# Linear attention and two gated layers on one core: idle-time products in the first batch, a second numerator buffer, split denominators, and output tiles shared between two engines

## The chip, the cores and the metric

The kernel runs on one core of a Trainium2 chip. The metric is the device time of one execution in microseconds (us), so smaller is better. Engines are named as in the profile: PE is TensorE (PEld its weight loads), DVE VectorE, ACT ScalarE, POOL GpSimd, SP SyncE, which here only issues DMAs. Each runs its own list of instructions in order and waits on semaphores for the others.

## What is computed

Inputs are 8 batches of 8 heads with 576 tokens and 64 dimensions. Attention is linear, with a feature map made of two exponentials; two token-wise layers follow.

```python
def phi(x):
    proj = np.einsum('bhsd,df->bhsf', x, w_phi)                 # 64 -> 128
    proj = proj - np.max(np.abs(proj), axis=-1, keepdims=True)
    return np.concatenate([np.exp(proj), np.exp(-proj)], axis=-1)
q_p, k_p = (phi(q), phi(k))
kv = np.einsum('bhsf,bhsd->bhfd', k_p, v)
z = np.sum(k_p, axis=2)
x = np.einsum('bhsf,bhfd->bhsd', q_p, kv) / (np.einsum('bhsf,bhf->bhs', q_p, z)[..., None] + 1e-06)
...
k = np.maximum(xk @ w_k, 0.0)          # xk, xr: x mixed with the token before, 512 -> 1024
y = 1.0 / (1.0 + np.exp(-(xr @ w_r))) * (k * k @ w_v)
...
h = np.maximum(y @ w_in, 0.0)          # 512 -> 1024, then a 3-tap convolution over tokens
out = (h * (1.0 / (1.0 + np.exp(-conv_out))) @ w_out)
```

## The kernel before

**Phase 1** does the attention and the first layer. Heads go in four pairs per batch, numbered p = 0 to 3. The first batch has nothing to run beside it: its order is written out in `first_attention_steps()`. From then on `iteration(batch)` weaves the attention of the next batch into the first layer's products of this one (tiles K, R, V in `psm`, three products for one at full precision, from a high and a low part of both operands). The steps of a pair, which every engine walks through in the same order and takes its own share of, are:

- `G` and `F`: PE projects keys into `ps1` and queries into `ps0` or `psm` (p even or odd); DVE then takes the key maxima and subtracts them (lines 948 to 961).
- `QT`: DVE transposes the projected queries and reduces them to partial maxima `q_part` (lines 966 to 973). `M`: PE turns them (line 640), DVE spreads them to `max_blocks` (977 to 985). `PICK`: PE subtracts them, ACT takes the four exponentials `q_exp` (line 837).
- `EK`, `EL`: ACT takes the exponentials of the keys (826, 830). `KV0`, `KV1`: PE sums keys by values, 9 float32 products each with 65 or 130 columns; ACT copies them to `kvz` (856).
- `DEN`, `NUM`: PE forms denominators and numerators. For pairs 0 and 1 ACT copies the denominators to `den_rows` (861) and the numerators to `num` (871). The denominators go through DMAs: out to `den_parts`, inverted by DVE on 9 columns (991, 994), stored to `den_scr`, read back to `den` by all partitions. `DV`: DVE multiplies `num` by `den` into `x` (1000). For pairs 2 and 3 (`WIDE` = 2) PE writes the denominator on all rows, ACT copies both to `num_first` and `den_first` (865, 866), and DVE inverts and multiplies half the tokens at a time (`D0`, `D1`, lines 1006 and 1009).
- `SH`, `SL`: one of ten weight pieces is rounded by ACT (line 820), and POOL takes what is left of it (line 554), a DMA having loaded it into `diff`, `mix` or `gate`. `XK`, `HK`, `LK`: DVE mixes tokens and splits the result for the first K tiles (1026 to 1053).

There is one `num` buffer, so `copy_num` of pair 1 waits until DVE has used that of pair 0 (`await_x`), and PE's projection of queries for pair 3, which goes over the same bank in PSUM, waits for `copy_num` of pair 1 (`await_q_psum`).

At the start, before data is there, PE runs `keep_warm(WARM_FIRST)`: 7 products of the identity with itself, written to an unused part of `ps1`. The step `WARM`, which does the same with `WARM` products, exists but no list contains it.

**Phase 2** does the second layer, batch by batch, two batches making a round c with half 0 and 1. PE makes 8 hidden tiles in `psh` (24 products each, 288 columns a product), then output tiles of 128 tokens by 512 columns: tiles 0 to 3 in `pso` (96 products for a batch), and after half 1 a tile 4 with the last 64 tokens of both batches, in the bank `psh[:, 1, 1]` (24 products). ACT scales each by 0.5 into `rows` (line 1254), and SP stores them (1172 to 1176). The semaphore `rows_ready` counts ACT's copies; PE and SP wait on it. At the end SP waits for all stores.

## Time and profile before

| | us |
|---|---|
| median of 3 timed runs | 1289.95 (1288.88 to 1289.97) |
| profiled execution | 1286.36 |
| its span in the profile | 1284.6 |
| PE busy | 1265.4 (99% of the span) |
| DVE, ACT, POOL busy | 816.4, 563.1, 142.8 |

Times in the rows count from the start of the span. A matmul in float32 shows as two records. A number in brackets is the idle time of that engine before the row, with what ended it. The granted TensorE clock stands as a share of full speed: 1.00 is 2.4 GHz, 0.50 is 1.2 GHz.

### The profile page before, as it was taken

Reading aid. Unit: us, or ns where it says so; the run is one execution under the profiler, and the core shown is the slowest. Engines: PE = TensorE matmul, PEld = TensorE weight load, DVE = VectorE, ACT = ScalarE, POOL = GpSimd, SP = SyncE. Lnnn points to the kernel's source line nnn. Section 1 sums busy time; section 2 is a strip of 40 time slices with the busy share of each in tenths; the row PEclk is TensorE's granted clock in tenths of the full one; section 3 lists DMA queues with packets and bytes.
Section 4 is the critical chain, followed back from the end, with each engine's and each line's share of the span. In section 5 each row is a group of like instructions: output and inputs, shape, how many; then the busy total and the mean of one; then the engine's idle time right before and its main releaser. Section 6 shows DMA issues by size and latency. Waiting matters only on the chain.

```text
span 1284.6 us, 23638 instructions
## 1 busy us (share of the span) xinstructions
PE 1265.4 (99%) x9506; PEld 1081.3 (84%) x9506; DVE 816.4 (64%) x1334; ACT 563.1 (44%) x1072; POOL 142.8 (11%) x137
## 2 busy tenths in 40 slices
PE   8889999999999999999999999999999999999998
PEld 6668887888788879788878878999899898898996
DVE  6788576576566766667657666546484583672852
ACT  4653634525434354353443544454344353352441
POOL 2512111102111211121111211000000000000000
PEclk8999999999999999999999999999999999999999
DMA  5512211221222222222131220422102102012001
GB/s 163 163 40 74 65 49 47 83 68 31 79 59 60 61 57 59 69 59 59 41 88 39 60 78 12 134 70 68 70 1 79 48 23 78 1 70 79 1 34 41
DMA packets 91540, 79.03 MB, mean 62 GB/s; under 512 B 61864, under 2 KB 70184, under 8 KB 90408
## 3 DMA queue, kind: packets, MB, share of 16 engines
q1 hardware_dynamic: 91272, 77.46, 19.9%
q8 instruction: 76, 1.25, 0.4%
q14 instruction: 32, 0.26, 0.1%
q10 hardware_dynamic: 160, 0.07, 0.0%
HBM read 58.21 MB, written 19.01 MB: 60 GB/s over the span
## 4 chain that ended last, share of the span: by engine, by line
PE 90%; DVE 3%; issue 3%; DMA 2%; ACT 1%; SPq 0%; ACTq 0%; DVEq 0%
PE psm L574 36%; PE ps L574 22%; PE psh L1197 6%; PE psh L1198 6%; PE psh L1196 6%; PE pso L1198 5%; PE pso L1196 5%; PE pso L1197 5%; PE ps L686 1%; DMA den<-den_scr 1%; ACT k_signs L826 1%; DMA den_scr<-den_cols 1%; DVE q_part L969 0%; DMA phi<-in_w_phi 0%; DVE mix L1034 0%
## 5 line engine op out<-in xcount | busy, mean ns | idle before, releaser
L574 PE MATMUL psm<-xy_hi,wk_hi 128*128 128x288 f32 x512 | 156.4, 306 | 6.6 <-DVE xy_lo L1053 3.9
L574 PE MATMUL psm<-k_hi,wv_hi 128*128 128x288 f32 x512 | 153.8, 300 | 0.0
L1198 PE MATMUL psh<-xy_hi,win_lo 128*128 128x288 f32 x512 | 151.3, 296 | 0.0
L1196 PE MATMUL psh<-xy_hi,win_hi 128*128 128x288 f32 x512 | 151.3, 296 | 0.0
L1197 PE MATMUL psh<-xy_lo,win_hi 128*128 128x288 f32 x512 | 151.3, 296 | 0.0
L574 PE MATMUL psm<-xy_lo,wk_hi 128*128 128x288 f32 x512 | 151.1, 295 | 0.0
L574 PE MATMUL psm<-k_lo,wv_hi 128*128 128x288 f32 x512 | 150.9, 295 | 0.0
L574 PE MATMUL psm<-k_hi,wv_lo 128*128 128x288 f32 x512 | 150.8, 295 | 0.0
L574 PE MATMUL psm<-xy_hi,wk_lo 128*128 128x288 f32 x512 | 150.7, 294 | 0.0
L1320 DVE SCALAR_TENSOR_TENSOR conv<-h,taps,conv 128x576 f32<-128x576 f32 x64 | 52.1, 814 | 138.8 <-ACT conv L1275 138.8
L562 POOL TENSOR_TENSOR z_pairs<-k_signs 128x512 f32<-128x512 f32 x56 | 73.2, 1307 | 601.7 <-ACT k_signs L826 597.7
L1058 DVE TENSOR_TENSOR k_lo<-square,k_hi 128x288 fp32r<-128x288 f32 x128 | 76.1, 617 | 62.4 <-ACT square L881 61.7
L826 ACT ACTIVATE k_signs<-k_signs 128x1152 f32<-128x1152 f32 x32 | 37.2, 1164 | 156.3 <-issue 138.8
L574 PEld LDWEIGHTS psm<-xy_hi,wk_hi 128*128 128x128 f32 x512 | 96.1, 188 | 10.9 <-ACT relu L876 4.0
L1198 PE MATMUL pso<-wk_hi,g_lo 128*128 128x512 f32 x256 | 101.3, 396 | 0.0
L1196 PE MATMUL pso<-wk_hi,g_hi 128*128 128x512 f32 x256 | 101.3, 396 | 0.0
L1197 PE MATMUL pso<-wk_lo,g_hi 128*128 128x512 f32 x256 | 101.2, 395 | 0.0
L574 PE MATMUL ps<-q_exp,kvz 128*64 128x512 f32 (+2 forms) x960 | 100.1, 415 | 0.0
L574 PEld LDWEIGHTS psm<-k_hi,wv_hi 128*128 128x128 f32 x512 | 96.2, 188 | 1.8
L1197 PEld LDWEIGHTS psh<-xy_lo,win_hi 128*128 128x128 f32 x512 | 96.3, 188 | 0.3
L1196 PEld LDWEIGHTS psh<-xy_hi,win_hi 128*128 128x128 f32 x512 | 96.1, 188 | 0.3
L574 PEld LDWEIGHTS psm<-xy_lo,wk_hi 128*128 128x128 f32 x512 | 96.3, 188 | 0.0
(147 smaller groups left out, 2830.2 us busy)
## 6 DMA issues: line engine op xcount, KB each, us to landing
k_in<-in_k SPq DMA_DIRECT2D x32, 320.0 KB, 3.3
v_nat<-in_v SPq DMA_DIRECT2D x32, 320.0 KB, 3.6
q_in<-in_q SPq DMA_DIRECT2D x32, 288.0 KB, 3.1
y_scr<-y SPq DMA_DIRECT2D x64, 144.0 KB, 2.5
y<-y_scr SPq DMA_DIRECT2D x8, 1152.0 KB, 5.8
den<-den_scr SPq DMA_DIRECT2D x60, 144.0 KB, 3.0
out<-rows SPq DMA_DIRECT2D x32, 256.0 KB, 2.0
stage<-in_moe_w_in SPq DMA_DIRECT2D x4, 512.0 KB, 4.0
```

The lines of the kernel that those rows point to most:

```text
L562: nc.gpsimd.tensor_tensor(z_pairs[:], tiles[:, 0], tiles[:, 1], ALU.add).then_inc(z_paired, 1)
L574: return nc.tensor.matmul(o, lhsT, rhs, start=first, stop=last, skip_group_check=True)
L686: last = nc.tensor.matmul(sums_back()[:, i, :], kvt[:, i, :], ident[:], start=True, stop=True, is_transpose=True, skip_group_check=True)
L826: nc.scalar.activation(k_exp, k_shift, ACT.Exp).then_inc(k_exp_ready, 1)
L1058: nc.vector.tensor_tensor(k2_lo[:, i, :], square[:, i % 2, :], k2_hi[:, i, :].bitcast(F32), ALU.subtract).then_inc(k2_lo_ready, 1)
L1196: nc.tensor.matmul(o, wh, xh, start=first, stop=False, skip_group_check=True)
L1197: nc.tensor.matmul(o, wh, xl, start=False, stop=False, skip_group_check=True)
L1198: return nc.tensor.matmul(o, wl, xh, start=False, stop=last, skip_group_check=True)
L1320: nc.vector.scalar_tensor_tensor(out=conv[:, j % 2, :], in0=h[:, hidden(c, half, j) % 3, 0:S], scalar=taps[:, 0, j:j + 1], in1=conv[:, j % ...
```

## The change

In the first batch, `WARM_FIRST` goes from 7 to 8, and a step `WARM` with 4 products is put ahead of `KV0` of pair 0. The numerators of pair 1 of the first batch go to `square`, a buffer of the first layer, so that their copy doesn't wait for `x`. `copy_wide` copies the first half of the denominators, then the numerators, then the second half. In phase 2, DVE takes the output tiles 1 and 3 (a new `copy_rows`), ACT keeps 0, 2 and 4, and `rows_ready` becomes `even_rows` and `odd_rows`. In the last round only, tile 4 is computed, copied and stored as two halves of 256 columns, each in a bank of its own.

```diff
-WARM_FIRST, WARM = 7, 6
+WARM_FIRST, WARM = 8, 4
...
-    steps = [("G", 0), ("F", 0), ("EK", 0), ("F", 1), ("QT", 0), ("KV0", 0), ("M", 0)] + hi()
+    steps = [("G", 0), ("F", 0), ("EK", 0), ("F", 1), ("QT", 0), ("WARM", 0), ("KV0", 0), ("M", 0)] + hi()
...
+    def numerator(p, a):
+
+        return square[:].rearrange("p i s -> p (i s)") if (p, a) == (1, 0) else num[:]
...
+            nc.scalar.activation(den_first[:, p - WIDE, 0:HALF], q_cols(1, p, a)[:, 0:HALF], ACT.Copy, bias=1e-6).then_inc(first_den, 1)
             nc.scalar.activation(num_first[:, p - WIDE, :], q_cols(0, p, a), ACT.Copy).then_inc(num_copied, 1)
-            nc.scalar.activation(den_first[:, p - WIDE, :], q_cols(1, p, a), ACT.Copy, bias=1e-6).then_inc(first_den, 1)
+            nc.scalar.activation(den_first[:, p - WIDE, HALF:S], q_cols(1, p, a)[:, HALF:S], ACT.Copy, bias=1e-6).then_inc(first_den, 1)
...
-            await_x(act, p, a)
-            nc.scalar.activation(num[:], q_cols(0, p, a), ACT.Copy).then_inc(num_copied, 1)
+            if (p, a) != (1, 0):
+                await_x(act, p, a)
+            nc.scalar.activation(numerator(p, a), q_cols(0, p, a), ACT.Copy).then_inc(num_copied, 1)
...
-            dve.wait_ge(first_den, own + 1)
+            dve.wait_ge(first_den, 2 * own + n + 1)
...
+    def await_all_rows(eng, c, half):
+
+        eng.wait_ge(even_rows, 5 * c + 2 * half)
+        eng.wait_ge(odd_rows, 4 * c + 2 * half)
+
+    def last_columns(c):
+
+        halves = slice(0, DM // 2), slice(DM // 2, DM)
+        return halves if c == TWOS - 1 else (slice(0, DM),)
...
-                for j in range(FT):
-                    last = out_part(0, 4, j)
-                last.then_inc(out_done, 1)
+                for n, cols in enumerate(last_columns(c)):
+                    for j in range(FT):
+                        last = out_part(0, 4, j, cols, n)
+                    last.then_inc(out_done, 1)
...
-            for t in range(4 + half):
+            for t in range(0, 4 + half, 2):
                 copy_rows(c, half, t)
...
+            for t in (1, 3):
+                copy_rows(c, half, t)
```

PE in the first batch, pair 0, before: query projections of pair 1 (`psm`), then `KV0`, then `M`.

```order
L574 MATMUL psm<-q_in,phi 128x64 [waits shared_bank] x2
L574 MATMUL ps<-v_nat,k_signs 128x65 [waits k_exp_ready,v_loaded]
L574 MATMUL ps<-v_nat,k_signs 128x65 x7
L574 MATMUL ps<-v_nat,k_signs 128x130
L640 MATMUL ps<-ident,q_part 128x128 [waits k_tail_shifted,q_part_ready]
```

The same place on PE with the change (the line numbers are those of the changed kernel):

```order
L578 MATMUL psm<-q_in,phi 128x64 [waits shared_bank] x2
L578 MATMUL ps<-ident 128x128 [waits k_shifted]
L578 MATMUL ps<-ident 128x128 x3
L578 MATMUL ps<-v_nat,k_signs 128x65 [waits k_exp_ready,v_loaded]
L578 MATMUL ps<-v_nat,k_signs 128x65 x7
L578 MATMUL ps<-v_nat,k_signs 128x130
L644 MATMUL ps<-ident,q_part 128x128 [waits k_tail_shifted,q_part_ready]
```

Four products of the identity stand between the projections and `KV0`.

ACT in the first batch, before, from the denominators of pair 1 to the exponential `EL` of pair 2:

```order
L861 ACTIVATE den_rows<-psm 128x576 [waits den_spread,attended]
L871 ACTIVATE num<-psm 128x576 [waits x_ready,attended]
L830 ACTIVATE k_signs<-k_signs 128x1152 [waits k_exp_ready]
L820 ACTIVATE wv_hi<-diff 128x1024 [waits piece_loaded0]
L820 ACTIVATE wv_hi<-mix 128x1024 [waits piece_loaded1]
```

The same place with the change:

```order
L865 ACTIVATE den_rows<-psm 128x576 [waits den_spread,attended]
L877 ACTIVATE square<-psm 128x576 [waits attended]
L834 ACTIVATE k_signs<-k_signs 128x1152 [waits k_exp_ready]
L824 ACTIVATE wv_hi<-diff 128x1024 [waits piece_loaded0]
L824 ACTIVATE wv_hi<-mix 128x1024 [waits piece_loaded1]
```

The copy has another target and no longer waits for `x_ready`; what stands behind it is the same.

ACT at the very end of the program, before:

```order
L1254 ACTIVATE rows<-pso 128x512 [waits stored0,out_done]
L1254 ACTIVATE rows<-pso 128x512 [waits stored1,out_done]
L1254 ACTIVATE rows<-pso 128x512 [waits stored2,out_done]
L1254 ACTIVATE rows<-pso 128x512 [waits stored3,out_done]
L1254 ACTIVATE rows<-psh 128x512 [waits stored4,out_done]
```

And with the change:

```order
L1279 ACTIVATE rows<-pso 128x512 [waits out_done,stored0]
L1279 ACTIVATE rows<-pso 128x512 [waits out_done,stored2]
L1279 ACTIVATE rows<-psh 128x256 [waits out_done,stored4]
L1279 ACTIVATE rows<-psh 128x256 [waits out_done]
```

Tiles 1 and 3 have left ACT for DVE, and the last tile's copy is in two parts of 256 columns.

## Rows read from the trace of the kernel before

**Rows 1.** Windows: us, busy by engine (instructions), granted PE clock, DMA share, GB/s.

```profile
17.93:28.17 10.24, 10.20 (x54) 6.33 (x55) 9.60 (x15) 4.77 (x7) 3.69 (x2) 0.50 0.45 136
28.17:1280.00 1251.83, 1240.56 (x9379) 1063.76 (x9376) 794.58 (x1301) 552.12 (x1058) 133.32 (x119) 1.00 0.20 59
```

**Rows 2.** Timeline of PE, 2 to 30 us: start, us, engine, line, what.

```profile
2.11 3.36 PE L574 MATMUL ps<-ident 128*128 128x128 f32 x14 [2.11 <-POOL ident L538]
6.08 2.80 PE L574 MATMUL ps<-phi,k_in 64*128 64x128 f32 x18 [0.61 <-DMA phi<-in_w_phi]
8.81 2.87 PE L574 MATMUL ps<-q_in,phi 64*128 64x512 f32 x8
...
12.03 1.79 PE L574 MATMUL psm<-q_in,phi 64*128 64x512 f32 x8
13.74 2.28 PE L574 MATMUL ps<-v_nat,k_signs 128*128 128x65 f32 x18
17.03 0.33 PE L640 MATMUL ps<-ident,q_part 128*128 128x128 f32 x1 [1.01 <-DVE q_part L973]
17.20 3.46 PE L574 MATMUL ps<-v_nat,k_signs 128*128 128x65 f32 x18
20.45 1.62 PE L574 MATMUL ps<-max_blocks,pick 128*128 128x512 f32 x4
...
24.53 4.94 PE L574 MATMUL ps<-q_exp,kvz 128*1 128x64 f32 x32
29.41 2.28 PE L574 MATMUL ps<-v_nat,k_signs 128*128 128x65 f32 x18
```

**Rows 3.** Timeline of PE, 31 to 46 us.

```profile
31.52 0.39 PE L574 MATMUL ps<-phi,k_in 128*128 128x128 f32 x2
...
38.97 3.25 PE L574 MATMUL psm<-q_exp,kvz 128*1 128x64 f32 x32 [0.15 <-ACT q_exp L837]
...
45.69 0.49 PE L574 MATMUL psm<-phi,k_in 128*128 128x128 f32 x2 [1.26 <-ACT num L871]
```

**Rows 4.** Timeline of ACT, 26 to 46 us.

```profile
26.70 1.16 ACT L826 ACTIVATE k_signs<-k_signs 128x1152 f32<-128x1152 f32 x1 [1.37 <-issue]
...
35.86 0.39 ACT L856 ACTIVATE kvz<-ps 128x260 f32<-128x260 f32 x1 [2.21 <-PE ps L574]
...
44.99 0.65 ACT L871 ACTIVATE num<-psm 128x576 f32<-128x576 f32 x1 [2.07 <-DVE x L1000]
```

**Rows 5.** Timeline of POOL, first and last of the pairs of pieces that DVE meets.

```profile
16.89 2.36 POOL L554 TENSOR_TENSOR wk_lo<-mix,wk_hi 128x1024 fp32r<-128x1024 f32 x1
...
50.05 2.38 POOL L554 TENSOR_TENSOR wv_lo<-mix,wv_hi 128x1024 fp32r<-128x1024 f32 x1
```

**Rows 6.** Timeline of DVE at the same places, and at the first K tiles.

```profile
17.72 1.57 DVE L979 CAST q_max_split<-q_max 128x32 fp32r<-128x32 f32 x1
...
50.80 1.68 DVE L973 COPY q_part<-q_part 128x64 f32<-128x64 f32 x1
...
71.16 1.95 DVE L1006 RECIPROCAL den_first<-den_first 128x288 f32<-128x288 f32 x1 [0.24 <-ACT den_first L866]
```

**Rows 7.** Timeline of PE, first product behind the second part of the mixed tokens.

```profile
77.60 0.37 PE L574 MATMUL psm<-xy_hi,wk_hi 128*128 128x288 f32 x1 [2.73 <-DVE xy_lo L1053]
```

**Rows 8.** Waits of DVE in phase 2: total us, times, longest.

```profile
DVE conv L1320 <- ACT conv L1275: 138.8, 16, 20.7
```

**Rows 9.** Timeline of ACT in phase 2: copies behind hidden tiles of 24 products each.

```profile
928.58 0.66 ACT L1273 ACTIVATE h<-psh 128x576 f32<-128x576 f32 x1 [1.74 <-PE psh L1198]
...
931.78 0.66 ACT L1273 ACTIVATE h<-psh 128x576 f32<-128x576 f32 x1 [1.16 <-PE psh L1198]
```

**Rows 10.** Timeline of the last tile: its first and last product, and its copy.

```profile
1274.76 0.40 PE L1196 MATMUL psh<-wk_hi,g_hi 128*128 128x512 f32 x1
...
1280.13 0.40 PE L1198 MATMUL psh<-wk_hi,g_lo 128*128 128x512 f32 x1
1280.57 0.60 ACT L1254 ACTIVATE rows<-psh 128x512 f32<-128x512 f32 x1 [5.00 <-PE psh L1198]
```

More of the change, by code:

```diff
@@ L1152, in token_tiles, with await_rows @@
         return c * TILES + (4 * half + n)
+    def await_rows(eng, c, half, t):
+        eng.wait_ge((even_rows, odd_rows)[t % 2], c * (4 + (t + 1) % 2) + 2 * half + t // 2 + 1)
+    def await_all_rows(eng, c, half):
[4 more added lines that the diff above has]
+        return halves if c == TWOS - 1 else (slice(0, DM),)
     def y_tiles(c, half, n):
@@ L1162, in two, with o_bank @@
         return cols.rearrange("p (b s) -> p b s", s=HALF)
-    def o_bank(t):
-        return pso[:, t, :] if t < 4 else psh[:, 1, 1, :]
+    def o_bank(t, n=0):
+        return pso[:, t, :] if t < 4 else psh[:, 1, 1 - n, :]
     def sync(sp):
@@ L1170, in store @@
             for t in range(4):
-                sp.wait_ge(rows_ready, token_tiles(c, half, t + 1))
+                await_rows(sp, c, half, t)
                 sp.dma_start(out[c * 2 + half][P * t:P * t + P, :], rows[:, t, :]).then_inc(stored[t], 16)
             if half:
-                sp.wait_ge(rows_ready, token_tiles(c, 1, 5))
-                sp.dma_start(out[c * 2 + 1][4 * P:S, :], rows[0:TAIL, 4, :]).then_inc(stored[4], 16)
-                sp.dma_start(out[c * 2][4 * P:S, :], rows[TAIL:P, 4, :]).then_inc(stored[4], 16)
+                for n, cols in enumerate(last_columns(c)):
+                    await_rows(sp, c, 1, 4 + 2 * n)
+                    sp.dma_start(out[c * 2 + 1][4 * P:S, cols], rows[0:TAIL, 4, cols]).then_inc(stored[4], 16)
+                    sp.dma_start(out[c * 2][4 * P:S, cols], rows[TAIL:P, 4, cols]).then_inc(stored[4], 16)
         def load_y(b):
@@ L1188, in sync @@
         store(TWOS - 1, 1)
-        for s in stored:
+        for s in stored[0:4]:
             sp.wait_ge(s, 16 * B)
+        sp.wait_ge(stored[4], 16 * B + 32)
     def tensor(pe):
@@ L1198, in three, with out_part @@
             return nc.tensor.matmul(o, wl, xh, start=False, stop=last, skip_group_check=True)
-        def out_part(at, t, j):
+        def out_part(at, t, j, cols=slice(0, DM), n=0):
             tok = slice(at + P * t, at + P * t + P)
-            return three(o_bank(t), (g_hi[:, j, tok], g_lo[:, j, tok]), (wout_hi[:, j, :], wout_lo[:, j, :]), j == 0, j == FT - 1)
+            return three(o_bank(t, n)[:, cols], (g_hi[:, j, tok], g_lo[:, j, tok]), (wout_hi[:, j, cols], wout_lo[:, j, cols]), j == 0, j == FT - 1)
         def batch(c, half):
@@ L1221, in batch @@
             else:
-                pe.wait_ge(rows_ready, token_tiles(c, half, 0))
+                await_all_rows(pe, c, half)
             for j in range(FT):
@@ L1231, in batch @@
                 pe.wait_ge(h_ready, hidden(c, half, FT))
-                for j in range(FT):
-                    last = out_part(0, 4, j)
-                last.then_inc(out_done, 1)
+                for n, cols in enumerate(last_columns(c)):
+                    for j in range(FT):
+                        last = out_part(0, 4, j, cols, n)
+                    last.then_inc(out_done, 1)
         batch(0, 0)
@@ L1253, in copy_rows @@
                 act.wait_ge(stored[t], 16)
-            nc.scalar.activation(rows[:, t, :], o_bank(t), ACT.Copy, scale=0.5).then_inc(rows_ready, 1)
+            for n, cols in enumerate(last_columns(c) if t == 4 else (slice(0, DM),)):
+                act.wait_ge(out_done, token_tiles(c, half, t + 1 + n))
+                nc.scalar.activation(rows[:, t, cols], o_bank(t, n)[:, cols], ACT.Copy, scale=0.5).then_inc(even_rows, 1)
         act.wait_ge(taps_loaded, 48)
@@ L1297, in split_y, with copy_rows @@
                 nc.vector.tensor_tensor(both.y_part(f, lo=True), both.y_cols(f), both.y_part(f).bitcast(F32), ALU.subtract).then_inc(y_lo_ready, 1)
+        def copy_rows(c, half, t):
+            dve.wait_ge(out_done, token_tiles(c, half, t + 1))
+            if c > 0:
+                dve.wait_ge(stored[t], c * 32 + 16 * half)
+            elif half:
+                dve.wait_ge(stored[t], 16)
+            nc.vector.tensor_scalar(rows[:, t, :], o_bank(t), 0.5, None, ALU.mult).then_inc(odd_rows, 1)
         for side in (0, S + 1):
```

10 lines of the change are left out of this document (5 added, 5 removed).

## The prediction, made before the changed kernel ran

> **What bounds the kernel now.** I read the windows first. From 28.17 to 1280 us PE is busy 1240.56 of 1251.83 us at full clock, so there the time is PE's own work, and no edit here takes any of it away. Before that, PE spends 10.24 us at half clock, 17.93 to 28.17 [rows 1]. So three places are left: the first batch, where four engines wait for each other, the wait of 2.73 us that ends it [rows 7], and what follows the last product [rows 10].
>
> In the first batch I followed the chain of waits backward from 77.60, where PE waits for the mixed tokens. It is DVE's work almost without a gap (the longest is the 0.24 us ahead of 71.16) back to `x` of pair 1. That one waits for the DMA of its inverse, which DVE takes up behind the copy to `q_part` that ends at 52.48 [rows 6]. That copy hangs on the query projections of pair 3, which PE began at 45.69 after waiting 1.26 us for the numerators of pair 1; ACT had stood idle 2.07 us before copying them [rows 3, 4]. Whatever moves 45.69 forward moves 77.60 forward, and with it all that PE does afterwards.
>
> **Sizes of the warm-up products.** Seven at the start take 3.36 us, 0.48 each, at the speed at which the first projections ran (2.87 us against 1.79 for the same eight records at full clock later) [rows 2]. A product of this shape at full clock is thus between 0.48 / 2 = 0.24 and the 0.39 us of the one with 128 columns at 31.52 [rows 3]; I take 0.31. The eighth at the start ends at 2.11 + 3.36 + 0.48 = 5.95, ahead of the 6.08 at which `phi` lets PE begin: it is free.
>
> **The four products ahead of `KV0`** cost 4 x 0.31 = 1.24 us (1.0 to 1.6). Before, `KV0` ran from 13.74 to 16.02, then PE stood 1.01 us until DVE's `q_part` [rows 2]. Now `KV0` ends at about 17.26 and `M` begins some 0.25 us later than 17.03. Behind `M` DVE casts the maxima, and that cast, 0.19 us or so of work, took 1.57 and ended at 19.29, just as POOL's piece ended at 19.25 [rows 5, 6]. The delay vanishes in that wait (up to about 1 us), so the products cost nothing in themselves as long as PE then is at full clock. If it is not, `KV1` takes 3.46 us from about 17.45 and ends later than the cast's chain, and `PICK` comes 0.3 us later than 20.45 [rows 2].
>
> **What they may bring is the clock.** It fell at 17.93, right after the idle 1.01 us and a stretch of products with 65 columns, and PE's work in the half-clock stretch took longer: `KV1` 3.46 against 2.28, `DEN` and `NUM` 4.94 against 3.25 us [rows 2, 3]. With that idle time filled by dense products, I expect it to stay at full. Then: `PICK` still waits for DVE's `max_blocks`, so it starts near 20.4, but by the same ratio of 1.5 takes about 1.1 instead of 1.62; `q_exp` comes 0.5 us earlier, and `DEN` and `NUM` run from 24.0 to 27.3. `KV0` of pair 1 then waits for the exponential that ended at 27.86 before [rows 4], now perhaps 0.3 earlier, for DVE loses less waiting for the keys. So `KV0` starts at 27.6 instead of 29.41: **1.8 us**. Bounds: 1.5 if that exponential does not move, 0 if the clock falls as before. From there to 45.69 each step hangs on the projections of pair 2, and I carry the 1.8 us through.
>
> The Trainium skill, "TensorE: Matmul & The Clock Gate", section "Why this matters for your kernels", ties a fall of the clock to long idle gaps between bursts. By it this idle time would not count, four products would change nothing, and the sum would be that of the first rival. The rows show a fall after 1.01 us, so I do not follow it, but it keeps that rival high.
>
> **The second numerator buffer.** ACT no longer waits for `x` of pair 0. The copy can follow `den_rows` at once, and PE's projections of pair 3 follow `KV0` of pair 2: `DEN` and `NUM` end at 38.97 + 3.25 = 42.2, `KV0` takes 2.28 [rows 2, 3] and ends at 44.45. They start 45.69 - 44.45 = **1.24 us** earlier. On ACT everything behind the copy moves by the idle 2.07 us, less a hand-over: about 1.9. That includes the two roundings that feed POOL, and POOL's piece at 50.05 ended at 52.43, where DVE's copy to `q_part` (50.80 + 1.68 = 52.48, of which 0.2 is work) had been held [rows 5, 6]. The copy could otherwise have started 1.24 earlier; now POOL ends at 50.5 and frees it 1.9 us earlier, which adds **0.7** (0 if the pieces are late from DMA). What is late next is PE's own work: nothing shorter than the exponential of pair 2's queries, which moves with the rest.
>
> That DVE is held for the whole POOL instruction is what the Trainium skill says too, "SBUF — State Buffer", section "SBUF: two separate sides". By it alone the 0.7 stands; without it the term would be 0.
>
> **Denominators in halves.** DVE's reciprocal at 71.16 had waited 0.24 us for the whole copy [rows 6]; the first half alone comes first now: **0.2 us**. The price is one more ACT instruction twice: 0.39 us for 260 columns against 0.65 for 576 [rows 4] means two halves of 0.4 instead of one of 0.65, of which 0.05 to 0.15 us lands on the exponential `EL` behind it in pair 3. DVE's chain, not PE, sets the end there, so it costs 0.
>
> **Rows on two engines.** PE never waits in phase 2, and DVE is idle 138.8 us there in 16 places, up to 20.7 us, each time while PE makes output tiles [rows 8]. A copy by DVE of 512 columns costs under 1 us inside that idle time. Behind DVE's new wait stand the next batch's convolutions, which need a hidden tile that PE begins only after the output tiles. ACT's first hidden copy comes 3.2 us after them. Both waits for two semaphores are met long before. Gain and cost: 0.
>
> **Last tile in halves.** 23 steps from 1274.76 to 1280.13 give 0.233 us for a product of 512 columns [rows 10]; two hidden copies 3.20 us apart give 0.133 for 288 [rows 9]. Both are nearly in proportion to the columns, so 256 columns should take 0.117 to 0.120: 48 x 0.118 = 5.7 against 24 x 0.233 = 5.6, a cost of 0.1 (bounds 0 and, if 0.133 is what a weight load allows at least, 48 x 0.133 - 5.6 = 0.8). After the last product ACT copies 256 columns instead of 512: 0.39 against 0.60, 0.2 saved. The last two stores carry half of the bytes; I give that 0.1 (0 to 0.4). Together **0.2** (-0.6 to +0.6).
>
> **Sum.** 1.8 + 1.24 + 0.7 + 0.2 + 0.2 = 4.1 us. Against the profiled execution that is 1286.36 - 4.1 = 1282.2, with a span of 1280.5. The median of the timed runs stands 3.6 us above the profiled execution, for which the profile has no reason; I keep this distance: 1289.95 - 4.1 = 1285.8.
>
> **Rivals.**
> 1. The clock falls in spite of the products. Half clock came after a stretch in which PE was mostly busy, so filling 1 us may not be enough. Then the 1.8 is gone and 0.3 is lost at `PICK`: 4.1 - 1.8 - 0.3 = 2.0, so 1288.0.
> 2. The clock stays up at 17.93 and falls a few us later, in the gaps that a faster PE leaves: 0.6 us before `PICK`, over 1 us before `M` of pair 1. Then the half-clock stretch covers `DEN`, `NUM` and the sums of pair 1, which PE's chain carries fully. By the ratio 4.94 / 3.25 = 1.52, a stretch of 10.24 us loses 10.24 x (1 - 1 / 1.52) = 3.5 us: 1289.95 - 4.1 + 3.5 = 1289.3. It decides for slower from 4.1 / 0.34 = 12 us of half clock on PE's chain; two such stretches, 20.5 us, cost 7.0 and give 1292.8. Against it: after 28.17 the clock stayed full over a wait of 1.26 us [rows 1, 3]. The same page of the Trainium skill, section "Part 1: The HAM clock gate", says that the switch is not tied to the kernel's start and that one kernel shows it at different places from run to run; by it, this rival holds in some executions.
> 3. The clock comes up earlier at the start, since the eighth product fills 0.5 of the 0.61 us before the first keys [rows 2]. The first query projections took 2.87 us where 1.79 would do, and the key maxima, exponentials and POOL follow them: at most 1.1 more, and 0.9 after DVE's own work, so 1284.9.
> 4. The halves of the last tile are held by their weight loads: 0.8 instead of 0.1, 1286.5.
>
> **Chances.** My forecast 0.50; rival 1 0.25; rival 2 0.08, half of it slower than before; rival 3 0.09; rival 4 0.08. 0.2%, or 2.6 us, is about what a measurement of this kernel can tell from no change; faster by that means under 1287.4. The forecast is there in nine of ten cases, rival 1 in one of five, rivals 3 and 4 nearly always: 0.45 + 0.05 + 0.09 + 0.07 = 0.66, I say 0.65. Slower by as much is only rival 2's long form, 0.04. The rest, 0.31, is the same. The range takes in rivals 3, 4 and 1 with their bounds and leaves out rival 2: 1284.2 to 1288.9.
>
> **What the changed profile would show.** A granted clock of 1.00 through 17.9 to 28.2, `KV1` at 2.3 us, `DEN` and `NUM` from about 24.0; the projections of pair 3 near 42.7 with no idle time for ACT's copy; the copy to `q_part` of pair 3 done near 48.7; the product that stood at 77.60 at 73.8 or so, still behind DVE; phase 2 unchanged in length, with no wait of PE; 48 last products in 5.6 to 5.8 us and the last copy at 0.39. I am wrong if the clock shows 0.50 anywhere after 12 us, if DMAs of the pieces hold ACT back, or if 77.60 moves by less than what its causes moved.

## The result: 7 us faster, more than the range allowed

| | before | changed |
|---|---|---|
| median of 5 timed runs, us | 1289.97 (1288.88 to 1292.05) | 1282.81 (1281.61 to 1283.21) |
| profiled execution, us | 1286.36 | 1282.67 |
| its span, us | 1284.6 | 1280.9 |

The ratio is 0.9941, with a 95% interval of 0.9927 to 0.9956. The forecast was 1285.8 with a range of 1284.2 to 1288.9, so the time lies outside it, on the fast side. From profile to profile the kernel gained 3.7 us, close to the 4.1 of the sum; from median to median it gained 7.2, and in three repetitions 6.4, 7.0 and 8.2. Before stands 3.6 us above its own profile in the median, the changed kernel 0.1. That distance turned out to be the case's main question. (Two executions that were disturbed as a whole, with 1741 and 3126 us, are left out of all numbers.)

**The clock.** The windows of the changed kernel (us, then busy time of PE, PEld, DVE, ACT and POOL with instructions, granted PE clock, DMA share, GB/s):

```profile
18.47:25.30 6.83, 6.41 (x39) 3.66 (x41) 6.33 (x11) 3.42 (x6) 1.50 (x1) 0.52 0.65 204
73.08:76.50 3.42, 2.79 (x12) 2.82 (x13) 3.32 (x6) 1.63 (x5) 0.00 (x0) 0.54 0.02 5
855.00:1270.00 415.00, 415.00 (x2491) 377.15 (x2490) 259.53 (x376) 163.48 (x248) 0.00 (x0) 1.00 0.13 44
```

Against [rows 1] the clock still falls in the first batch, for 6.8 us instead of 10.2, and a second, short stretch at half clock has appeared right behind the wait at 73.7. Phase 2 is as it was: PE is busy in all of 415.00 us.

**The first batch.** The timeline of PE (start, us, engine, line, what, and in brackets the idle time before it and what ended it):

```profile
6.38 1.58 PE L578 MATMUL ps<-phi,k_in 64*128 64x128 f32 x18 [0.80 <-DMA phi<-in_w_phi]
...
15.40 0.33 PE L644 MATMUL ps<-ident,q_part 128*128 128x128 f32 x1 [0.49 <-DVE q_part L979]
15.57 2.18 PE L578 MATMUL ps<-v_nat,k_signs 128*128 128x65 f32 x18
18.85 1.62 PE L578 MATMUL ps<-max_blocks,pick 128*128 128x512 f32 x4 [1.10 <-DVE max_blocks L991]
...
40.12 2.26 PE L578 MATMUL ps<-v_nat,k_signs 128*128 128x65 f32 x18
42.21 0.39 PE L578 MATMUL psm<-phi,k_in 128*128 128x128 f32 x2
...
73.71 0.58 PE L578 MATMUL psm<-xy_hi,wk_hi 128*128 128x288 f32 x1 [2.78 <-DVE xy_lo L1059]
```

The first row is the first key projections: 1.58 us instead of the 2.80 of [rows 2], so the clock was up before them. The next two are `M` and `KV1`, which stood at 17.03 and 17.20. `KV1` now takes 2.18 us instead of 3.46, but PE then waits 1.10 us for DVE before `PICK`, and the clock falls in that wait. The projections of pair 3 at 42.21 follow `KV0` without idle time, where before PE waited 1.26 us at 45.69 [rows 3]. The product that stood at 77.60 [rows 7] is at 73.71, still behind DVE. ACT (the copy of pair 1's numerators, and one of the roundings), POOL and DVE at the places of [rows 4 to 6]:

```profile
40.76 0.65 ACT L877 ACTIVATE square<-psm 128x576 f32<-128x576 f32 x1
...
43.74 1.06 ACT L824 ACTIVATE wv_hi<-mix 128x1024 fp32r<-128x1024 f32 x1 [0.34 <-DMA mix<-in_moe_w_v]
```

```profile
45.82 2.39 POOL L558 TENSOR_TENSOR wv_lo<-mix,wv_hi 128x1024 fp32r<-128x1024 f32 x1
```

```profile
47.21 1.05 DVE L979 COPY q_part<-q_part 128x64 f32<-128x64 f32 x1
```

The copy has lost its wait of 2.07 us. A rounding waits 0.34 us for its piece, a wait that takes back a little of it. POOL's piece ends at 48.21 instead of 52.43, and DVE's copy ends with it, at 48.26 instead of 52.48.

**The last tile**, PE's first and last product, ACT's last copy and SP's last store, and above them DVE's copy of output tile 3:

```profile
1271.73 0.69 DVE L1331 TENSOR_SCALAR rows<-pso 128x512 f32<-128x512 f32 x1 [0.71 <-PE pso L1220]
```

```profile
1271.53 0.28 PE L1218 MATMUL psh<-wk_hi,g_hi 128*128 128x256 f32 x1
...
1277.10 0.27 PE L1220 MATMUL psh<-wk_hi,g_lo 128*128 128x256 f32 x1
1277.41 0.38 ACT L1279 ACTIVATE rows<-psh 128x256 f32<-128x256 f32 x1 [2.37 <-PE psh L1220]
...
1278.33 0.60 SPq L1197 DMA_DIRECT2D out<-rows  x1
```

47 steps take 5.57 us, against 23 steps in 5.37 in [rows 10].

**Where 3.7 us went, profile to profile.** From the starts of four products in both timelines: `M` of pair 0, `M` of pair 2, the first product of the K tiles behind the second part of the mixed tokens (called `K` below), and the last product.

| stretch, us | before | changed | gain |
|---|---|---|---|
| start to `M` of pair 0 | 17.03 | 15.40 | 1.63 |
| to `M` of pair 2 | 21.49 | 21.08 | 0.41 |
| to `K` | 39.08 | 37.23 | 1.85 |
| to the last product | 1202.53 | 1203.39 | -0.86 |
| to the end of the span | 4.47 | 3.80 | 0.67 |

The third and the fifth line are the second buffer and the tail. The first can't be credited to the change: in nine profiles of this study with seven products at the start, as before, `M` of pair 0 began between 14.40 and 19.61, and in the eleven with eight between 14.87 and 17.45. The fourth contains the new half-clock stretch behind `K`, and 0.2 us of the last tile's products.

### The profile page after: what moved, and what is told of

Its sections match the earlier page's. It is cut to its first block, busy times and chain, and to the rows that moved or that the text cites. A ratio compares the mean times of both kernels' runs of the same rounds, so it can differ in the third digit from the quotient of the medians.

```text
span 1280.9 us, 23723 instructions
## 1 busy us (share of the span) xinstructions
PE 1263.5 (99%) x9540; PEld 1082.4 (85%) x9540; DVE 828.3 (65%) x1350; ACT 553.8 (43%) x1059; POOL 142.8 (11%) x137
## 4 chain that ended last, share of the span: by engine, by line
PE 92%; DVE 4%; issue 2%; ACT 1%; DMA 1%; ACTq 0%; SPq 0%; DVEq 0%
PE psm L578 38%; PE ps L578 21%; PE psh L1219 6%; PE psh L1218 6%; PE psh L1220 6%; PE pso L1218 5%; PE pso L1220 5%; PE pso L1219 5%; PE ps L690 1%; ACT k_signs L830 1%; DVE q_part L975 0%; DMA phi<-in_w_phi 0%; DVE q_turn L972 0%; PE ps L644 0%; DVE mix L1040 0%
## 5 line engine op out<-in xcount | busy, mean ns | idle before, releaser
L578 PEld LDWEIGHTS psm<-xy_hi,wk_lo 128*128 128x128 f32 x512 | 96.8, 189 | 0.0
```

The source lines that it names most:

```text
L578: return nc.tensor.matmul(o, lhsT, rhs, start=first, stop=last, skip_group_check=True)
```

## Is the profile of before typical?

The first question was whether the parts give more than I had thought, or whether the profile of before was a lucky execution. Four kernels on one chip: before once more, and three parts alone.

**Before, again** (no edit).

> The kernel before, run as if it were a change. Theory A: the profiled execution of before (1286.4 us) was one in which the half-clock stretch was short, and the timed ones have a longer or a second one. Then the mean granted clock of the timed runs here is below 0.996, each with a span near 1288, and a run with 0.996 is near 1286. Theory B: the 3.6 us have nothing to do with the clock; then clocks of 0.996 go with spans near 1288. Ratio 1.000 either way.

Measured: 1287.33 us (12 runs), beside 1288.68 (30 runs) of the same kernel in the comparison, ratio 0.9993 (0.9975 to 1.0011). So two sets of the same kernel differ by 1.3 us in the median without a cause in the code; a difference of that size between two sets proves nothing. Its profile took 1286.5 us with the mean granted clock at 0.992. The first profile of before had one stretch at half clock, 10.24 us [rows 1], which is 1 - 0.5 x 10.24 / 1284.6 = 0.996. The new one has three (windows, columns as above):

```profile
12.00:30.00 18.00, 16.52 (x115) 12.00 (x115) 13.49 (x19) 10.85 (x14) 8.28 (x4) 0.81 0.42 121
42.00:55.00 13.00, 12.85 (x65) 9.63 (x67) 7.02 (x11) 6.54 (x9) 5.94 (x3) 0.61 0.41 117
70.00:84.00 14.00, 10.80 (x68) 10.62 (x69) 11.58 (x18) 8.06 (x19) 4.23 (x4) 0.88 0.00 1
```

A clock of 0.81 over 18.00 us is 2 x 0.19 x 18.00 = 6.8 us at half clock; the others make 10.1 and 3.4. The longest is this one:

```profile
43.08:53.32 10.24, 10.14 (x55) 8.30 (x53) 5.37 (x9) 5.05 (x8) 4.75 (x2) 0.50 0.46 134
```

And the timeline of PE there:

```profile
42.05 0.49 PE L574 MATMUL psm<-phi,k_in 128*128 128x128 f32 x2 [1.53 <-ACT num L871]
42.47 2.58 PE L574 MATMUL psm<-q_in,phi 64*128 64x512 f32 x8
44.98 4.21 PE L574 MATMUL ps<-v_nat,k_signs 128*128 128x65 f32 x18
...
52.93 4.28 PE L574 MATMUL ps<-q_exp,kvz 128*64 128x64 f32 x32
```

This is the wait for the numerators of pair 1, 1.53 us, and 1 us behind it the clock is down. The nine sums of keys by values take 4.21 us instead of the 2.28 of [rows 2]. In the first profile of before the clock stayed full behind the same wait (1.26 us, [rows 3]). From `M` of pair 2 to `K` it is 42.43 us here, against 39.08 there: this stretch costs **3.4 us**.

How often? Every timed run lists its mean granted clock. Of 125 runs of before in all series, 75 are at 0.993 or below, which is some 17 us of half clock or more, with a median of 1289.4 us. The 20 runs at 0.996 have 1285.3. In between the time rises with the half clock: medians of 1287.3 us at 0.993 (12 runs), 1288.5 at 0.992 (25) and 1290.5 at 0.991 (37). The profile I worked from has the 0.996 of the minority, and the median over all is 1288.8.

That profile was not simply a fast one, though. The new one has the second fall and still took only 1286.50 us, the least of the 25 runs at 0.992: its `M` of pair 0 begins at 14.52 instead of 17.03, and from there to `M` of pair 2 it needs 20.07 us instead of 21.49. What the first execution was spared at the second fall it had lost before.

**The warm-up products alone.**

```diff
-WARM_FIRST, WARM = 7, 6
+WARM_FIRST, WARM = 8, 4
-... ("F", 1), ("QT", 0), ("KV0", 0), ("M", 0)] + hi()
+... ("F", 1), ("QT", 0), ("WARM", 0), ("KV0", 0), ("M", 0)] + hi()
```

> Before with the 8 products at the start and the step of 4 products ahead of the first key-value sums, nothing else of the change. Theory A: this part holds most of what I missed: 1289.97 - 4 to 5 = 1285 to 1286 us, with a mean clock at or above 0.996. Theory B (the missing part lies in phase 2 or in the second buffer): 1.8 us at most, 1288.2 or more.

Measured: 1286.05 us (12 runs), 0.9985 (0.9971 to 0.9999), and 3 of 12 runs at 0.993 or below. In its profile, 1287.95 us, the clock stays full from 12 to 30 us, then falls behind the wait for the numerators (6.8 us at half clock) and again ahead of 84 us. As in rival 2 a fall comes later instead of not at all, but at the wait that I had held against that rival.

**The second numerator buffer alone.**

```diff
-            await_x(act, p, a)
-            nc.scalar.activation(num[:], q_cols(0, p, a), ACT.Copy)...
+            if (p, a) != (1, 0):
+                await_x(act, p, a)
+            nc.scalar.activation(numerator(p, a), q_cols(0, p, a), ACT.Copy)...
```

> Before with the second buffer for the numerators of pair 1 alone. By the sum of the prediction: 1.24 + 0.7 = 1.9 us faster, 1288.0; the projections of pair 3 start near 44.5 instead of 45.7. If the missing gain is here, 4 us or more.

Measured: 1283.35 us (7 runs), 0.9964 (0.9944 to 0.9983), the largest effect of any part, 5.3 us below the 1288.68 of before in the medians and 4.6 by the ratio, and no run of 7 at 0.993 or below. Its window from 42 to 55 us, and then that of the first profile of before:

```profile
42.00:55.00 13.00, 11.87 (x97) 8.43 (x93) 11.00 (x17) 8.40 (x13) 7.19 (x3) 1.00 0.60 179
```

```profile
42.00:55.00 13.00, 10.12 (x89) 7.87 (x87) 8.88 (x14) 7.86 (x12) 5.84 (x4) 1.00 0.57 168
```

Read them, and the one of before again above, by the count of PE's instructions: 97, 89 and 65 in the same 13 us. PE is busiest in the last, 12.85 us, and gets least done, since each product takes longer. `M` of pair 2 to `K` is 37.34 us here: 1.7 below the 39.08 without a fall, 5.1 below the 42.43 with one.

**All of the change in phase 2 alone** (output tiles 1 and 3 on DVE, the last tile in halves; lines as in the diff of the change).

> Before with the whole change of phase 2 (output tiles 1 and 3 on VectorE, last tile in halves), nothing in phase 1. By the two profiles, the time from the last product to the end fell from 4.4 to 3.8 us and the halves cost 0.1: 0.5 us faster, 1289.5. The rival that the missing gain is in phase 2: 3 us or more faster, and the length of phase 2 in the profile then changes.

Measured: 1287.34 us (12 runs), 0.9992 (0.9976 to 1.0008), not to be told from no change, with 7 of 12 runs at 0.993 or below. The end of its span is clear, though: 3.79 us from the start of the last product to the end, against 4.47. ACT's last copy:

```profile
1278.62 0.38 ACT L1273 ACTIVATE rows<-psh 128x256 f32<-128x256 f32 x1 [2.37 <-PE psh L1214]
```

## Is it the clock, or the wait itself?

The theory by now: in most executions of before the clock falls behind PE's wait for pair 1's numerators, and the second buffer is worth so much since it takes away that occasion. The rival: the buffer lets other engines go on earlier by all of 5 us, and the clock only goes along. The kernel that tells them apart keeps the wait and fills it.

**The changed kernel, again** (no edit), for the comparison on this chip.

> The changed kernel again, as the measure for the others of this series. Both theories: 1282 to 1284 us, ratio 0.994 to 0.997. By theory C (below) its mean clocks are 0.996 and more, never the 0.991 or 0.992 that most executions of before show.

Measured: 1282.4 us (11 runs) beside 1288.81, ratio 0.9959 (0.9945 to 0.9974). Nine of the runs are between 1281.7 and 1283.5. Its profile has 3.4 us of half clock at 50 to 54 us, behind a wait for DVE's keys, and `M` of pair 2 to `K` takes 39.32 us for it: the buffer does not shut out every fall there.

**Before, with four identity products in the gap.**

```diff
-WARM_FIRST, WARM = 7, 6
+WARM_FIRST, WARM = 7, 4
-            steps += hi() + [("F", p + 1)] + lo() + ...
+            steps += hi() + ([("WARM", p)] if p + 2 == PAIRS else []) + [("F", p + 1)] + lo() + ...
```

> Before with 4 products of the identity (1.2 us) put into the idle time in which TensorE waits for the numerators of pair 1; the wait itself stays. Theory C: the second buffer is worth more than its 1.9 us because its idle time lets the clock fall for 10 us in most executions. Then filling it makes the clocks of 0.991 and 0.992 rare, and the median falls by 1.5 to 3 us although no wait is gone. Theory D: the buffer's 5 us are all waiting time, or luck of the series; then this is 0 or slower, and clocks stay at 0.992.

Measured: 1284.94 us (12 runs), 0.9976 (0.9959 to 0.9992), and no run of 12 at 0.993 or below, where the runs of before beside it have 18 of 34; by luck alone that would be a matter of 1 in 1300. PE's timeline:

```profile
40.25 1.05 PE L574 MATMUL ps<-ident 128*128 128x128 f32 x8
...
41.86 0.49 PE L574 MATMUL psm<-phi,k_in 128*128 128x128 f32 x2 [0.55 <-ACT num L871]
...
43.99 2.28 PE L574 MATMUL ps<-v_nat,k_signs 128*128 128x65 f32 x18
```

The projections still start only when ACT has copied the numerators (41.86, where it was 42.05). Only PE's idle time is different, 0.55 us instead of 1.53. `KV0` behind them takes 2.28 us. The clock now falls later in this profile, near 49.7 us behind a wait for DVE's keys, and for 3.4 us instead of 10.2, and `M` of pair 2 to `K` takes 41.02 us. In the medians, four useless products bring 3.9 us (3.1 by the ratio) of the 5.3 (4.6) that the buffer brings. They bring no engine forward, so that part is the clock; what is left, 1.4 or 1.5 us, fits the 1.7 of the wait. The sizes are loose: the intervals reach from 1.0 to 5.3 us for the fill and from 2.2 to 7.2 for the buffer, and the two were measured in different series. That the clock is the larger part is shown by the counts and the medians; the two profiles differ by 1.5 us only.

All 20 profiles of the study, sorted by what the clock did between `M` of pair 2 and `K`, say the same:

| at half clock, 42 to 70 us | one buffer: `M` of pair 2 to `K`, us | two buffers |
|---|---|---|
| none | 2, 39.08 and 38.95 | 11, 37.23 to 37.89 |
| 3.4 us | 2, 40.99 and 41.02 | 1, 39.32 |
| 6.8 us | 1, 41.43 | none |
| 10.2 us | 2, 42.43 and 42.54 | none |
| 13.5 us | 1, 44.52 | none |

Row by row the buffer is worth 1.7 us, and it moves the profiles into the first row. In seven of the eight with one buffer the wait for the numerators isn't filled. Behind four of these waits the clock falls (1.53, 1.56, 1.67 and 1.83 us), behind three it doesn't (1.03, 1.26 and 1.46 us).

**The changed kernel with one numerator buffer.**

```diff
-            if (p, a) != (1, 0):
-                await_x(act, p, a)
-            nc.scalar.activation(numerator(p, a), ...
+            await_x(act, p, a)
+            nc.scalar.activation(num[:], ...
```

> The changed kernel with one numerator buffer again. Theory C: 1.9 us of wait and in many executions a half-clock stretch come back, 3.5 to 5 us slower than the changed kernel, clocks of 0.994 and less. Theory D without luck: 1.9 us slower.

Measured: 1286.95 us (12 runs), 0.9989 (0.9973 to 1.0006), 4.6 us above the changed kernel beside it. Two of 12 runs are at 0.993 or below and eight at 0.995 or below, where the changed kernel has two of 11 at 0.995 or below, and `M` of pair 2 to `K` is back at 38.95 us in its profile, without a fall there. That profile also shows that eight products do not always bring the clock up early: the first query projections take 2.88 us, as in [rows 2], and `M` begins at 17.45.

```profile
9.19 2.88 PE L574 MATMUL ps<-q_in,phi 64*128 64x512 f32 x8
```

**The changed kernel without the warm-up products** (`WARM_FIRST` 7 and no step `WARM`).

> The changed kernel with 7 products at the start and without the step of 4. The prediction put 1.8 us on it, by a clock that stays full; the profile of the changed kernel shows half clock there all the same, only later and shorter. I now expect 0 to 1.5 us slower than the changed kernel, and every profile with a half-clock stretch that begins before 18 us.

Measured: 1282.87 us (12 runs), 0.9961 (0.9944 to 0.9978), beside 1282.4 with them; the difference of 0.5 us is not shown. No run is at 0.993 or below. So the buffer does that by itself. (Alone, the warm-up products gave 2.6 us, the buffer 5.3 and the tail 1.3, which makes 9.2, against 6.4 for all together. With 1.3 us between two sets of the same kernel that is no proof of an overlap, but an overlap is what the clock would give: both keep the same stretches from adding up.)

## What is left of the clock term

**A third time the changed kernel** (no edit).

> The changed kernel once more, in one series with a try to better it. 1282 to 1283 us.

Measured: 1282.24 us (8 runs), 0.9941 (0.9921 to 0.9961). This profile shows what my term of 1.8 us was about: the clock is full from 12 to 30 us.

```profile
12.00:30.00 18.00, 14.78 (x126) 10.89 (x124) 13.54 (x19) 11.45 (x15) 8.20 (x4) 1.00 0.39 120
```

```profile
15.13 0.33 PE L644 MATMUL ps<-ident,q_part 128*128 128x128 f32 x1 [0.51 <-DVE q_part L979]
...
18.56 0.93 PE L578 MATMUL ps<-max_blocks,pick 128*128 128x512 f32 x4 [1.09 <-DVE max_blocks L991]
...
22.06 0.30 PE L644 MATMUL psm<-ident,q_part 128*128 128x128 f32 x1 [1.48 <-DVE k_signs L957]
```

`PICK` takes 0.93 us instead of 1.62, as forecast, and PE waits 1.48 us for DVE's keys right behind. The stretches from `M` of pair 0 to `M` of pair 2 over all profiles of the study but that of a late start (below):

| at half clock, 14 to 30 us | profiles without the four products | with them |
|---|---|---|
| none | none | 6, 19.48 to 19.56 us |
| 6.8 us | 8, 20.01 to 20.59 us | 3, 21.08 to 21.62 us |
| 10.2 us | 2, 21.49 and 21.23 us | none |
| mean | 20.42 | 20.13 |

So the four products do keep the clock full in six of nine. But a full clock is worth only 0.7 us against the usual short stretch (19.5 against 20.2 us in the mean), which begins between 15 and 18 us; only against the longer one of the profile that I worked from it is 1.9. Where the clock falls in spite of them it falls later, in PE's wait for DVE, and costs about 1.2 more than the usual. The mean gain is **0.3 us**, and that is all that is left of the term. The products themselves cost nothing: from the query projections of pair 1 to `M` it is 5.40 us in this profile (9.73 to 15.13) and 5.43 in the second one of before (9.09 to 14.52), and the 0.25 us that I had put on `M` does not show. DVE sets the end as soon as PE is fast, as the waits of 1.09 and 1.48 us show.

**Filling the wait ahead of `K`, too.** In the changed kernel the clock falls behind the wait of 2.78 us at 73.71. Nine identity products were put there.

```diff
+        if batch == 0 and step == ("K-", 0, 2):
+            out.append(("WARM", 0))
-                    keep_warm(WARM)
+                    keep_warm(WARM if m is None else 9)
```

> The changed kernel with 9 products of the identity (2.6 us) put into the longest wait that is left, the 2.8 us before the first K tile's second part. Theory C: each idle time of 1 us or more in which the clock may fall costs in a part of the executions; in the profile of the changed kernel the clock was at half from 73.1 to 76.5 us, right behind this one. Filling it then takes 0.5 to 1.5 us off the median (1281.5) and no profile shows half clock there. Rival: the waits before the turned maxima of pairs 1 and 3 take the fall instead, or the products delay the K tile; then 0 or slower.

Measured: 1281.73 us (6 runs), 0.9939 (0.9916 to 0.9962), beside 1282.24. Its timeline and window:

```profile
69.94 2.17 PE L580 MATMUL ps<-ident 128*128 128x128 f32 x18
...
72.88 0.37 PE L580 MATMUL psm<-xy_hi,wk_hi 128*128 128x288 f32 x1 [0.77 <-DVE xy_lo L1061]
```

```profile
72.00:84.00 12.00, 11.23 (x97) 9.71 (x97) 10.43 (x22) 8.17 (x23) 0.07 (x1) 1.00 0.03 6
```

The first product behind the wait takes 0.37 us as in [rows 7], instead of 0.58, and the stretch has no half clock. In the profiles with and without a fall at this place the way from `K` to the last product differs by 0.6 to 2.1 us (1202.53 and 1202.76 in the two profiles with the fill, 1203.33 to 1204.59 in three of the changed kernel), but the medians differ by 0.5.

**The denominators in halves alone** (in before; the edits to `first_den` as in the diff of the change).

> Before with the denominators in halves alone. Prediction: 0.2 us, too small for the times; in the profile the reciprocal of the first half begins without waiting for ScalarE and the exponential behind the copies of pair 2 ends 0.05 to 0.15 us later. If more of what was missed lies here, 1 us or more.

Measured: 1288.81 us (12 runs), 1.001 (0.9991 to 1.0029): nothing. In the profile the reciprocal that waited 0.24 us [rows 6] no longer waits (77.65, and 66.89 in the changed kernel), as forecast. This profile, 1293.29 us, is the longest of the study, and the cause stands at its beginning:

```profile
12.53 3.15 PE L574 MATMUL psm<-q_in,phi 64*128 64x512 f32 x8
15.61 4.21 PE L574 MATMUL ps<-v_nat,k_signs 128*128 128x65 f32 x18
...
48.03 0.49 PE L574 MATMUL psm<-phi,k_in 128*128 128x128 f32 x2 [1.83 <-ACT num L872]
```

The same 8 and 18 records took 1.79 and 2.28 us in [rows 2]: here PE runs at half speed until past 28 us, and `M` of pair 0 begins at 19.61. This is a **late start**: the clock has not risen when the queries are projected. Runs of this kind show in the timed ones by a high mean clock with a long time: 6 of the 125 of before have 0.998 or more and 1290.0 to 1290.8 us. The sign misses those in which the clock falls later, as in this very execution (0.995): another 8 of the 125, with 0.994 or 0.995 and 1293 us or more, may be of this kind.

**Rows on two engines alone** (output tiles 1 and 3 on DVE, last tile whole).

> Before with output tiles 1 and 3 on VectorE, the last tile whole. Prediction: 0 us, no wait of TensorE in phase 2, and from the last product to the end 4.4 us as before; the difference to the run with all of the change in phase 2 is then what the halves give, 0.6 us.

Measured: 1290.49 us (12 runs), 1.0004 (0.9989 to 1.0018): nothing, as forecast, with 11 of 12 runs at 0.993 or below. Its last copy is that of [rows 10]:

```profile
1282.51 0.60 ACT L1272 ACTIVATE rows<-psh 128x512 f32<-128x512 f32 x1 [5.71 <-PE psh L1213]
```

## The eighth product, the four, and the fill once more

Four kernels with one comparison (12 runs, median 1289.73 us) take the changed kernel apart at its start.

**The changed kernel, a fourth time.**

> The changed kernel in the series of the two below. 1282 to 1283 us.

Measured: 1281.5 us (5 runs), 0.9940 (0.9927 to 0.9952). In its timeline `K` stands with 0.58 us, and the two products behind it at 0.44:

```profile
72.72 0.58 PE L578 MATMUL psm<-xy_hi,wk_hi 128*128 128x288 f32 x1 [2.77 <-DVE xy_lo L1059]
73.09 0.44 PE L578 MATMUL psm<-xy_lo,wk_hi 128*128 128x288 f32 x1
73.33 0.44 PE L578 MATMUL psm<-xy_hi,wk_lo 128*128 128x288 f32 x1
```

**Without the step of four products** (the list as in before, `WARM_FIRST` 8).

> The changed kernel with 8 products at the start but without the step of 4. If the step only moves the first fall of the clock a few us later, as the profiles show, this is within 1 us of the changed kernel, and its profile has a half-clock stretch that begins before 18 us. If the step is worth the 1.8 us of the prediction, 1284 us.

Measured: 1280.79 us (6 runs, 1280.09 to 1286.05), 0.9945 (0.9927 to 0.9963). The step that carried my largest term brings nothing here. Its window shows the short stretch at half clock that the profile just above does not have:

```profile
12.00:30.00 18.00, 16.55 (x117) 12.02 (x115) 13.58 (x18) 11.12 (x15) 7.92 (x4) 0.81 0.41 114
```

**Seven products at the start** (the step kept).

> The changed kernel with 7 products at the start, the step of 4 kept. If the eighth product makes the first rise of the clock come earlier in some executions, this is 0.3 to 1 us slower in the median and has more executions above 1284; if not, the same.

Measured: 1283.14 us (8 runs, 1281.31 to 1288.67), 0.9954 (0.9937 to 0.9971), 1.6 us above the fourth changed kernel and 0.9 above the third. The intervals overlap. What differs is the kind of the worst runs. Of the kernels with two buffers, those with seven products at the start have 5 of 27 runs with a mean clock of 0.999 or 1.0 and yet 1285.9 to 1288.7 us, late starts; those with eight have none of 58. By luck alone that would be a matter of 1 in 400; in the two series that have both kinds it is 4 of 20 against none of 27, 1 in 37, and the sign was chosen with the runs in view. So it is likely, but not shown, that the eighth product takes away a loss of some 5 us in about every fifth run, which a median hardly shows. It isn't free in every execution, as I had it: where `phi` is early, the keys begin at 5.37 or 5.39 us behind seven products (three profiles) and at 5.82 behind eight (four).

**The filled wait ahead of `K`, again.**

> The changed kernel with 9 products in the last long wait, again. If the 0.5 us of the first series is real, 0.3 to 1.5 us below the changed kernel of this series, with clocks of 0.999 and 1.000 in half of the runs; if it was chance, the same.

Measured: 1282.06 us (5 runs), 0.9940 (0.9926 to 0.9953), beside 1281.5. Both sets together, 11 runs, have a median of 1282.06, and the changed kernel's 29 runs have 1282.2. The fill keeps the clock up in both of its profiles (clock 1.0 over the span), and the time shows no gain from it.

**Without the step, again, and with the fill.** Two more, beside 11 runs of before with a median of 1288.51 us.

> The changed kernel without the step of four products, eight products at the start. The question is whether the step brings anything once the numerators have a second buffer. If it is worth nothing or a little less (the first set had 1280.8 us in the median, the changed kernel's 29 runs 1282.2), this one lies at 1280.5 to 1282. If the first set was luck, it lies at 1282 to 1283.5, since then the step keeps its 0.2 to 0.5 us. In both cases the first stretch at half clock should begin near 16 us and last 6 to 7 us, so that the mean clock is 0.997 at most in nearly all runs, and no run should show a late start (a mean clock of 0.998 or more and a time of 1285 or more).

Measured: 1280.97 us (6 runs, 1280.02 to 1281.6), 0.9941 (0.9922 to 0.996), all six at a mean clock of 0.997. From `M` of pair 0 to `M` of pair 2 it is 20.09 us.

> The same, and nine identity products in the wait ahead of the first K tiles' second part: the combination of the two edits that looked best. If the half clock behind that wait costs 0.7 to 2.1 us whenever it comes, the two together lie near 1280 us; if it comes seldom without the step (its one profile did not show it), the fill brings under 0.3 us and both kernels of this call agree within 0.5 us.

Measured: 1280.99 us (6 runs, 1279.96 to 1281.82), 0.994 (0.9919 to 0.9961). The fill brings nothing beside it. The 12 runs without the step have a median of 1281.0, the 29 of the changed kernel 1282.2; but by the ratios to before, 0.9945 and 0.9941 against 0.9959, 0.9941 and 0.9940, no difference is left. Leaving the step out costs nothing, and whether it gains 1 us is not shown.

## Why the prediction was wrong, and which parts held

**The step that failed** is the one that came last: "The median stands 3.6 us above the profiled execution, for which the profile has no reason; I keep this distance". The distance was for the most part the cost of falls of the clock that the timed executions have and the profiled one does not: 75 of 125 runs of before are at 0.993 or below, 4.1 us above those at 0.996, and between two profiles such a fall costs 3.4 us. The change removes its occasion: none of 24 repeated runs of the changed kernel, nor of the first 5, is at 0.993 or below. Filling the wait alone, with one buffer, took 3.9 us off the median. So the term of the second buffer, 1.9 us, measured 5.3 (4.6 by the ratio), and the distance that was carried on as a constant fell from 3.6 to 0.1. That the distance is exactly this one fall is not shown: the other profile of before has the fall and took 1286.50 us, by an earlier start.

**Luck.** Without the distance the sum would have given 1282.2, and the profiled execution took 1282.67; the product at 77.60 was forecast near 73.8 and came at 73.71. Neither bears the sum out. Of the 3.89 us by which that product moved, 1.63 lie ahead of `M` of pair 0, where the sum had nothing and where executions scatter by up to 5 us, and the clock term gave 0.41 instead of 1.8. Of the three signs of being wrong that I had named, two came: half clock after 12 us, and a DMA that held ACT back, by 0.34 us.

**Second buffer, 1.24 + 0.7 = 1.9 us.** The mechanism was right, step by step: no wait at the copy, the projections behind `KV0`, POOL and DVE free earlier. Measured against the same kind of execution it is 1.7 (39.08 to 37.34). Against the usual one it is 5.1 (42.43 to 37.34), and 5.3 in the medians. This term was mis-sized, by the clock: I had priced the wait of 1.26 us by its length, since the clock stayed full behind it in one execution. DVE's copy again took 1.05 us, of which 0.2 is work, and ended with POOL's piece; the Trainium skill, "SBUF — State Buffer", section "SBUF: two separate sides", agrees with that.

**The clock kept full, 1.8 us.** The effect is there in six of nine profiles, but the size is wrong. `PICK` took 0.93 us (forecast: 1.1) and `KV1` about 2.2 (2.3), and then PE waits 1.48 us for DVE's keys, a wait that the step left out. And the 10.24 us at half clock [rows 1] that it was measured against are as untypical as the rest of that execution; the usual 6.8 us cost 0.7. With the later falls counted the mean is 0.3 in the profiles, and the timed runs without the step show no loss.

**Rival 1**, a fall at the old place in spite of the products, is in none of the nine profiles with them. **Rival 2** came in short form in the changed kernel's own profile: the clock falls 3 us behind `M`, in the wait of 1.10 us ahead of `PICK`, and stays at half for 6.8 us. It had the right mechanism, a fall in a gap of PE that the chain carries fully, and a good price, 3.5 for 10.24 us. I set it only against the changed kernel and argued it away with one wait of 1.26 us in one execution; in its long form, behind that very wait, it was at work in before. **Rival 3** is right in kind, but it can't be laid to the eighth product: the first keys take 1.58 us in the changed kernel's profile, and 1.58 to 1.89 in five of the nine with seven products too. **Rival 4** is out: 47 steps in 5.57 us are 0.1185 each, in proportion to the columns as forecast.

**Tail, 0.2 us.** 0.67 gained behind the last product, 0.2 lost in the products: 0.5, within its bounds. The copy and its start give 0.35, as forecast or a little more, and the stores, from the last one's issue to the end, took 2.56 us instead of 2.86: 0.3 where I took 0.1.

**Denominators, rows on DVE: 0.2 and 0.** Neither shows in the medians. The wait of 0.24 us is gone, and from `M` of pair 2 to `K` the halves are worth 0.1 (37.23 against 37.34, and 38.95 against 39.08 with one buffer). DVE's copy of 512 columns takes 0.69 us, in idle time.

**Like with like.** Runs of before at a mean clock of 0.996 have 1285.3 us in the median, those of the changed kernel at the same clock 1282.9 (11 runs). The difference of 2.4 is 1.7 of the buffer, 0.5 of the tail and 0.2 that is not placed. The other 4 us or so of the gain are the stretches at half clock that before has more of.

**What stays open:** why the same wait is followed by a fall in some executions and not in others (the lengths of seven waits, 1.03 to 1.46 us without a fall and 1.53 to 1.83 with one, are too few to go by, and other waits of 1.48 us and of 2.8 us had none), and what decides when the clock first rises.

## What to carry to other kernels

Before a sum is made from a profile, compare the profiled execution's time and mean clock with those of the timed runs; if they differ by more than the runs scatter, find out what the profile lacks before carrying the distance on. A wait of PE of 1 to 2 us is worth more than its length when the clock falls behind it. To tell the two apart, fill the wait with products whose result nobody uses: what they bring is the clock, and what they don't bring is the wait.

## What the runs showed of the hardware that was not expected

- The clock can fall behind a wait of 1.53 us (behind 1.01 us in [rows 1, 2]) and stay at half for 10.24 us; with 1.05 us of products in that wait, the runs at 0.993 or below went from 18 of 34 in the same series (75 of 125 in all) to none of 12. The Trainium skill, "TensorE: Matmul & The Clock Gate", section "Why this matters for your kernels", ties a fall to long idle gaps; the gaps ahead of the falls in these profiles are 1.0 to 2.8 us, and the measurement decides.
- The same 10.2 us at half clock cost 3.4 us in one stretch and 1.9 in another, and 6.8 us there only 0.7: where DVE sets the end, a full clock only lengthens PE's waits.
- The mean clock of a run is no full account of its time: a late start doesn't show in it. In the profile of the kernel with denominators in halves the granted clock reads 1.00 from 0 to 28 us, while 8 records take 3.15 us instead of 1.79.
- Identity products of 128 columns in float32 take 0.24 to 0.26 us at full clock (2.17 us for nine, 1.05 for four), where I had taken 0.31.
